# Another order for ScalarE, VectorE and GpSimd behind the sixth attend: chunked attention followed by two feed-forward layers

## The reference

```python
q, k, v: (8, 8, 576, 64)          # batch, heads, sequence, head size
scores = scale * matmul(q_c, k_c.T)      # in chunks of 64 positions
attn = exp(scores - max(scores)); attn = attn / (sum(attn) + 1e-09)
x = matmul(attn, v_c)                    # -> (4608, 512)
xn = x / sqrt(mean(x * x) + 1e-06) * rms_g
x = (silu(xn @ w_gate) * (xn @ w_val)) @ w_out     # d_ff 1536
h = x @ w_in
out = (h * clip(h + 3, 0, 6) / 6) @ w_out2         # d_ff 2048
```

## Time and profile before

| what | value |
|---|---|
| median of 3 runs | 1644.12 us |
| lowest and highest | 1643.08 and 1645.68 us |
| the profiled execution, its own time | 1643.31 us |
| span of its trace | 1641.5 us |
| TensorE busy | 1602.5 us, 98% of the span |
| VectorE, ScalarE, GpSimd busy | 1048.4, 859.0, 797.8 us |
| mean granted clock of TensorE | 0.995 of full speed |

### The profile page before, as it was taken

The page is one execution under the profiler, slowest core; times in us unless marked ns, Lnnn a source line. Parts: engine busy times, 40 slices in busy tenths (PEclk is TensorE's granted clock), DMA queues, the critical chain, the costliest instruction groups (busy, mean ns, idle before and its releaser), DMA issues.

```text
span 1641.5 us, 29728 instructions
## 1 busy us (share of the span) xinstructions
PE 1602.5 (98%) x11332; PEld 1569.7 (96%) x11332; DVE 1048.4 (64%) x1436; ACT 859.0 (52%) x1341; POOL 797.8 (49%) x779
## 2 busy tenths in 40 slices
PE   6899999999999999999999999999999999999998
PEld 5698999999999999999999999999999999999998
DVE  5778878867755445755455776665666865455454
ACT  5576766755544444644444565554665654434432
POOL 2753443558866664523230377687675631231231
PEclk9899999999999999999999999999999999999999
DMA  9686876635565655989997856647648986676674
GB/s 175 151 197 152 200 192 168 174 117 173 166 231 189 210 193 204 370 313 313 311 312 281 297 206 232 239 173 254 217 175 299 373 265 200 218 228 212 212 229 118
DMA packets 335646, 366.88 MB, mean 223 GB/s; under 512 B 186256, under 2 KB 299152, under 8 KB 332304
## 3 DMA queue, kind: packets, MB, share of 16 engines
q1 hardware_dynamic: 319472, 334.16, 64.4%
q0 software_dynamic: 8800, 28.85, 5.2%
q10 hardware_dynamic: 7232, 1.97, 0.7%
HBM read 200.80 MB, written 164.10 MB: 222 GB/s over the span
## 4 chain that ended last, share of the span: by engine, by line
PE 85%; DMA 3%; DVE 3%; issue 3%; ACT 3%; POOL 2%; SPq 1%; ACTq 0%; DVEq 0%; POOLq 0%
PE bx L993 14%; PE by L993 14%; PE bx L994 13%; PE bx L995 13%; PE by L994 13%; PE by L995 13%; DMA hl_b<-h_scratch 1%; PE att L962 1%; DVE tx L1531 1%; PE att L918 1%; PE att L971 1%; PE att L941 1%; ACT tx L1179 1%; DMA v_first<-in_v_dram 1%; DMA h_scratch<-ht 1%
## 5 line engine op out<-in xcount | busy, mean ns | idle before, releaser
L993 PE MATMUL bx<-tx,wr 128*128 128x384 f32 x840 | 285.5, 340 | 6.5 <-DVE tx L1531 4.2
L993 PE MATMUL by<-tx,wr 128*128 128x384 f32 x840 | 285.8, 340 | 2.2 <-DVE vb L1557 1.5
L995 PE MATMUL bx<-tx,wr 128*128 128x384 f32 x840 | 281.3, 335 | 0.0
L994 PE MATMUL by<-tx,wr 128*128 128x384 f32 x840 | 281.3, 335 | 0.0
L995 PE MATMUL by<-tx,wr 128*128 128x384 f32 x840 | 281.2, 335 | 0.0
L994 PE MATMUL bx<-tx,wr 128*128 128x384 f32 x840 | 281.2, 335 | 0.0
L1583 DVE TENSOR_TENSOR hl_d<-hl_d 128x1536 fp32r<-128x1536 f32 x84 | 147.2, 1786 | 93.7 <-ACT hl_d L1280 93.5
L1903 POOL DMA_DIRECT2D out_dram<-ot x128 | 70.2, 556 | 248.8 <-DVE ot L1606 246.3
L1583 DVE TENSOR_TENSOR hl_b<-hl_b 128x1152 fp32r<-128x1152 f32 x84 | 119.1, 1433 | 107.2 <-ACT hl_b L1280 106.8
L1280 ACT ACTIVATE hl_d<-hl_d 128x1536 fp32r<-128x1536 f32 x84 | 123.1, 1485 | 114.6 <-DMA hl_d<-u_scratch 114.6
L993 PEld LDWEIGHTS bx<-tx,wr 128*128 128x128 f32 x840 | 158.2, 188 | 10.9 <-DVE tx L1531 5.7
(11 more groups left out here) (205 smaller groups left out, 3783.0 us busy)
## 6 DMA issues: line engine op xcount, KB each, us to landing
hl_d<-u_scratch SPq DMA_DIRECT2D x84, 768.0 KB, 4.4
hl_b<-h_scratch SPq DMA_DIRECT2D x84, 576.0 KB, 5.9
u_scratch<-ut SPq DMA_DIRECT2D x48, 576.0 KB, 3.7
h_scratch<-ht SPq DMA_DIRECT2D x36, 576.0 KB, 3.8
u_scratch<-ub SPq DMA_DIRECT2D x96, 192.0 KB, 3.1
u_scratch<-ub SPq DMA_DIRECT2D x48, 384.0 KB, 2.5
h_scratch<-vb SPq DMA_DIRECT2D x72, 192.0 KB, 3.2
h_scratch<-vb SPq DMA_DIRECT2D x36, 384.0 KB, 3.6
```

What stands on the lines that cost most here:

```text
L993: pe.matmul(dst, w_hi, m_hi, start=start, stop=False, skip_group_check=not opens)
L994: pe.matmul(dst, w_hi, m_lo, start=False, stop=False, skip_group_check=not opens)
L995: return pe.matmul(dst, w_lo, m_hi, start=False, stop=stop, skip_group_check=not opens)
```

## The change

Four lists (one of each engine but SyncE; GpSimd's by way of a table) are touched. On ScalarE the norm of chunk 4 and the copy of k for chunk 6 go ahead of the mean square of chunk 5; the norm of chunk 5 goes ahead of the second part of weight unit 1; the exponential and the copy of chunk 6 go ahead of the first early fill. On VectorE the fill of operand 0 (the first remainder) and the eviction of chunk 4 go ahead of the shift of chunk 6's scores. On GpSimd the second part of weight unit 2 moves from slot 2 to slot 5, behind the inverse norm of chunk 6. TensorE gets four instead of six dummy matmuls ahead of step 0. No other work is added or taken away.

```diff
-    LO_POOL_AT = {2: ((0, 2), (0, 2)), 3: ((0, 11), (0, 12)), 5: ((1, 13), (1, 13))}
+    LO_POOL_AT = {2: ((0, 2), (0, 5)), 3: ((0, 11), (0, 12)), 5: ((1, 13), (1, 13))}
...
-        keep_busy(6, att[:, AB, :])
+        keep_busy(4, att[:, AB, :])
...
+        norm_rows(S_FIRST - 2)
+        copy_k(S_FIRST)
         mean_square(S_FIRST - 1)
-        norm_rows(S_FIRST - 2)
         weight_hi(1, 0)
-        copy_k(S_FIRST)
+        norm_rows(S_FIRST - 1)
         weight_hi(1, 1)
-        norm_rows(S_FIRST - 1)
-        fill_hi_early(1)
         exponentials(S_FIRST)
         copy_probsT(S_FIRST)
+        fill_hi_early(1)
         fill_hi_early(2)
...
-        shift_scores(S_FIRST)
         fill_lo(0, 0)
         evict_x(S_FIRST - 2)
+        shift_scores(S_FIRST)
         evict_x(S_FIRST - 1)
```

## The result

| | before | after |
|---|---|---|
| median, 14 runs each | 1643.66 us | 1638.74 us |
| lowest and highest | 1637.84, 1646.80 | 1634.89, 1643.49 |
| the profiled execution, its own time | 1643.31 | 1638.90 |
| its span | 1641.5 | 1637.1 |

What follows compares the result with a forecast made beforehand. TensorE, 98% busy, bounds the kernel; chunk 6's transpose starting at 65.4 instead of 67.69 takes 2.3 us off 1643.31, giving 1641.0; from the median 1641.8, stated as 1641.7. Range 1640.0 to 1643.6, over all cases 1638.9 to 1644.4.

Steps and rivals of the forecast that it cites:

- What bounds the kernel: TensorE, busy 98% of the span: the change is worth what it moves the start of chunk 6's transpose at 67.69 us.
- The front part: Reordered ScalarE and VectorE work from chunk 4's norm to slot 2: slot 2 starts some 4.5 us sooner.
- The dummy matmuls: On TensorE between chunk 6's scores and slot 0, beside VectorE's fill: removing two costs nothing.
- Where the lead ends: At SyncE's unmoved transfers: chunk 6's attend not before 53.5 us, third sum on GpSimd at 58.2 behind the second x_scratch store.
- Turns at the port: GpSimd and VectorE operations exclude each other and the waiting one goes next: transpose of chunk 6 at 65.4 us.
- the tie at 58.1: VectorE's fill against GpSimd's third sum: same end either way; if wrong for both, one more fill, 1.4 us gain remains.
- The rival's half that no turn is given away: On GpSimd the inverse norm directly follows the first weight part: 3.1 us, up to 3.9; chance 0.30 with the clock case.
- The sum of 2.3 us: Chunk 6's transpose on TensorE starts at 65.4 us instead of 67.69.
- The clock: TensorE behind chunk 6's transpose: a piece at 1.2 GHz as before, 2.7 us better or worse at the ends.
- the second half of the first rival: TensorE's clock is back sooner: 2.3 + 2.7 = 5.0 us, so 1639.1; chance 0.30 with the case of no turn given away.
- the lead would be constant from 75 us on: Sign of a right forecast: from 75 us on a constant lead of 2.3 to 2.8 us.
- The rival of a whole lead of 4.5 us: The front's whole lead survives past the x_scratch store issued at 51.87 us: 1639.6 us; chance 0.06.

Runs made afterwards that it cites:

- e3: Changed kernel with six dummy matmuls ahead of step 0 in place of four; median 1638.95 us, ratio 0.9986 to the kernel before.
- e6: Changed kernel with the second x_scratch store issued one place earlier on SyncE; median 1637.77 us, ratio 0.9973 to the kernel before.
- e5: The changed kernel measured again, nothing altered; median 1638.39 us against 1642.57, ratio 0.9973 to the kernel before.
- e11: The changed kernel a third time, nothing altered, one execution for its profile; span 1638.3 us.
- e7: Changed kernel with VectorE's fill of operand 4 moved from slot 6 to slot 7; median 1640.69 us, ratio 0.9980 to the kernel before.
- e1: Kernel before with the GpSimd edit alone, weight unit 2's second part behind the inverse norm; median 1637.80 us against 1641.32, ratio 0.9988.
- e2: Changed kernel with the GpSimd edit undone, so front and dummy matmuls alone; median 1641.20 us against 1641.32, ratio 0.9998 to the kernel before.
- e8: Changed kernel with SyncE's list of loads and stores reordered; first run median 1636.80 us against 1642.57, ratio 0.9969 to the kernel before.

## Why the prediction was right in sign and short in size

**What bounds the kernel.** Right: the start of chunk 6's transpose collects what is won in front of it. Slot 2 had its lead in every kernel with the new front: over three profiles each it started at 55.0 us before and 49.1 after, and of these 5.8 us the transpose kept 2.4. The kernel with the front alone lost it to stalls of 1.59, 1.25, 2.25 and 3.00 us on TensorE.

**The front part.** Right in its lead, forecast as 4.5 us and measured as 4.2 in the first pair. The starts were late: the scores at 40.50 for 39.2, slot 0 at 42.62 for 41.6, slot 2 at 50.49 for 49 to 50.2. SyncE's row was later too, but only by 0.5 us (its first q load for chunk 8 at 37.25, not 36.79). The forecast also lacks a wait: chunk 4's transpose stood 1.03 us behind VectorE's eviction (`xr`, line 1525), not behind its norm, and the other profiles with the new front have that wait too (0.46 to 1.04 us). The dummy matmuls were costed at nothing; e3 shows 0.3 us at slot 0 and nothing behind it on the path, and leaves the time open.

**Where the lead ends.** Right: the sums of unit 2 at 51.5 for 51.1, the attend at 53.04 for 53.5, and the store's landing as the anchor. Its landing was forecast at 58.2 and came at 59.4, by the two deviations named (issued 0.6 us later, 0.6 us longer on its way). e6 shows that the transpose follows the store one for one.

**Turns at the port.** Right where a fill takes its turn behind the third sum and another in front of the inverse norm: forecast 7.2 us from the third sum to the transpose, measured 6.93 (e5) and 7.04 (e11), and 7.37 (e3) with a third turn. But the first profile took 6.19 us. The forecast played the tie at 58.1 both ways, with the sum or the fill waiting for the other; it did not price the third way, in which the fill is over before the sum can start. That term was too long by 1.0 us in this profile. The anchor was late by 1.2 us (59.47 for 58.2), and it is by luck that the two nearly cancel in a transpose at 65.66 for 65.4. The rival's half that no turn is given away falls with the rows: the inverse norm took 1.26 us in the changed kernel, and 0.55 in e7, where the fill was moved.

**The sum of 2.3 us.** The mean start of the transpose over three profiles each is 66.8 before and 64.4 after: 2.4 us. The third sum starts at 57.6 and 57.7 in the mean, so it is the distance that shrank. Against the first profile's 9.4 us, the e1 and e2 runs split it: 2.5 us for GpSimd's entry alone, 1.3 for the rest alone, together 2.4 to 3.2.

**The clock.** The forecast took a piece at half speed as before, with 2.7 us to either side. That size was too large: it cost 1.8 us in the first profile and 0.8 to 1.5 in three others. In the first pair the second half of the first rival came true: the clock stayed at 2.4 GHz behind the transpose and made 3.85 us of lead out of 2.0. But it is chance for both kernels (two in three each), so no part of the difference of the medians can be put on it by these runs.

**What stays open.** The medians moved by 4.9 and 4.2 us, with 2.6 us as the lower end of the first interval and 2.5 (0.9985 of 1642.57) of the second; what is located is 2.4 at chunk 6's transpose. So a change by over 0.2% came, which the forecast had given 0.36, and no mechanism that it named for that case is shown to be the reason. In the means of three profiles each the lead is 2.4 us at chunk 6, 2.8 at chunk 7, 1.5 at the last chunk and 3.5 at the end. From the last chunk's transpose to the end the fourteen profiles took between 1292.9 and 1299.9 us (the longest is e2's, the slowest of its twelve executions), with before between 1294.2 and 1298.0 and after between 1293.5 and 1294.3. Whether the change has a further effect in there, or three profiles of each just fell so, is not settled. That the lead would be constant from 75 us on, as forecast, is wrong in the first pair: it was 3.9 us at chunk 7, 3.2 from chunk 9 to 18, 2.4 at chunk 19, 2.8 at the last and 4.4 at the end. The rival of a whole lead of 4.5 us is excluded for the place where it was priced (e2), though its time, 1639.6, is near the measured one.

## What to carry to other kernels

Look for the last wait that collects an earlier lead before pricing that lead, and ask what its releaser waits for: here it was a store behind a full row of DMA issues, and of the 4 us that a reordered front gained, 1.3 got past it (e2), and those by another way, over fewer turns given to VectorE. A short operation that others wait for (0.55 us) belongs ahead of a long one (2.5 us) on an engine in order: that entry alone gave 2.5 us of distance here, and 2.0 us of time with an interval of 0.3 to 3.6. A lead measured early in a trace is not yet time: 4.6 us at chunk 6 (e8) were 1.6 us in the medians. Durations beside another engine's work hold waits; compare them with the same operation alone before adding them up.

## What was not expected of the hardware

Whether TensorE drops to 1.2 GHz behind a stall did not follow from the stall's length: 3.00 us (e2) and 1.94 us (e3) left it at 2.4 GHz, 1.96 us (e11) was followed by 1.2 GHz (mean granted clock 0.66 in the window from 64 to 68 us). Two executions of one kernel differ by up to 3.5 us in when the third sum starts (59.47 and 56.01) and by up to 3.8 us between the last chunk and the end, so that of one profile only distances over short stretches tell something at this size.
